# A delta-rule attention kernel: the look-ahead work of its first pass moved into the rounds of the second

## The chip, the cores and the metric

One core of a Trainium2 chip. The metric is the device time of the whole program in microseconds, lower is better. TensorE does matmuls into PSUM, VectorE (DVE) and ScalarE (ACT) move and combine tiles, GpSimd (POOL) works on SBUF tiles only, and SyncE (SP) issues most of the DMAs.

## The reference

Three stages follow each other: an attention with a running 40 x 40 state per head (4 batches, 8 heads, 768 tokens), a mixture of eight experts with one expert per token, and a dense layer. The change is in the first alone:

```python
for t in range(S):
    y[:, :, t] = einsum('bhd,bhde->bhe', rt, state)
    Sa = einsum('bhde,bhe->bhd', state, at)
    state = state * wt[:, :, None, :] - einsum('bhd,bhe->bhde', Sa, bt) + einsum('bhd,bhe->bhde', vt, kt)
```

## The kernel before

The attention works in chunks of C = 64 tokens. A step (or round) k takes one chunk of 8 pairs of heads; there are 24, twelve for one half of the batches and then twelve for the other, so the state is zero again after round 11. Within a chunk the effect of the a and b vectors on each other is a triangular matrix whose two 32 x 32 diagonal blocks are inverted; the lower left block (`off`) joins the halves later.

**First pass (24 steps).** For each step VectorE makes the decays of the chunk by two scans, `suf` backwards (L431) and `wq` forwards (L438) with a reciprocal between them (L436), and scales with them: `second` = b times suf (L445), `alpha` = a times wq (L446). TensorE makes from these the blocks (`g1`) and b turned to have time on the partitions (`bt`), each by `heads` (L764), 16 matmuls that the profile shows as 32 records. ScalarE copies the blocks to `off_all` and, negated, b to `btm_all` (L676 to L679). SP writes the blocks to memory in another order (L356) and loads them for the inversion (L294), with four steps in one group (GROUP), so 128 blocks of 32 x 32 lie on 128 partitions. Groups 0 and 1 are inverted by VectorE in halves of 16 (`invert_halves`, L130, behind step 11, AT_DVE), and the eight steps of these groups are then joined by small matmuls in steps 15 to 22 (AT_JOIN, L892 to L904). Groups 2 to 5 are inverted whole by GpSimd (`invert_blocks`, L109): two memsets, then for each of 31 columns j a product and a subtraction over (j+1)(31-j) elements per partition, each waiting for the one before.

**Second pass (24 rounds).** VectorE makes the same scans again (for k, the key) two rounds ahead, and `second` and `alpha` one round ahead. TensorE runs 17 groups by `heads` and one by `picks` per round inside a hardware loop (L916), each behind semaphores of what it reads: w (alpha with the state, and g2 with v), s (turned state), ktm, u, a part of the new state, z, m1, sa and sat, st (new state), m2, g2 of the next round, y. The banks are shared: w, z, sat and m2 lie in BA, s, m1 and y in BB, u, sa and g2 in BC, the key, the new state and the picks in BD. VectorE masks g2, m1 and m2 (L477), adds z to w (L517), scales the new state to `swt` (L534), takes y out of its bank (L452) and reduces the gate logits (L459). ScalarE takes out w, s, ktm, u, sa, sat, and prepares `off`, `btm`, `inv` (L708) for the next round. TensorE may write s only when y_out has read BB.

The order on each engine is written out by hand; each engine does its instructions in that order. SP's list per round is at L375 to L393. Around the loop stand warming matmuls (`warm`, L837). After the last round come the routing, the experts and the dense layer, which no edit touches.

Of the kernel before, what the change touches and what calls it, by code (L numbers as in the profile page):

```python
# [15 lines left out]
PARTS = 128  # L16
# [92 lines left out]
def invert_blocks(eng, sem, base, h, q, share):  # L109

    count = [0]
# [6 lines left out]
    link(eng.memset(flat, 0.0))  # L118
    link(eng.memset(flat[:, 0:B * B:B + 1], 1.0))
    for j in range(B - 1):  # L120
# [9 lines left out]
def invert_halves(eng, sem, h, q, share):  # L130

    count = [0]

    def link(ins):
        count[0] += 1
        ins.then_inc(sem, 1)
        eng.wait_ge(sem, count[0])

    def on_diagonal(t, i, j, rows_of, columns):
        first = t[:, B * i + j:B * i + j + 1]  # L140
        return bass.AP(first.tensor, first.offset, [first.ap[0], (HB * B + HB, 2 * BY_DVE), rows_of, columns])
    for j in range(HB - 1):
        n = HB - 1 - j
        part = share[:, 0:BY_DVE * 2 * (j + 1) * n].rearrange("q (d j t) -> q d j t", d=2 * BY_DVE, t=n)
        link(eng.tensor_tensor(part, on_diagonal(q, 0, j, (B, j + 1), (0, n)), on_diagonal(h, j, j + 1, (0, j + 1), (1, n)), ALU.mult))
        rest = on_diagonal(q, 0, j + 1, (B, j + 1), (1, n))
        link(eng.tensor_tensor(rest, rest, part, ALU.subtract))


HB = B // 2  # L150
HALVES_STEPS = 2 * (HB - 1)
INVERT_STEPS = 2 + 2 * (B - 1)
BLOCK_AT = B * B + B
BY_DVE, AT_DVE = 2, 11
JOINED = BY_DVE * GROUP
AT_JOIN = 15
BY_POOL = range(BY_DVE, GROUPS)


def attention(nc, inp, dram, keep):  # L160

    with ExitStack() as ctx:
# [3 lines left out]
        def ring(name, n, shape):  # L166
            return [m_.sb(f"{name}{s}", shape) for s in range(n)]
        W_COLS, A_COLS = HS * WIDE, HS * C
        t_in = ring("t_in", TR, [PARTS, W_COLS + 2 * A_COLS])
        restart = m_.sb("restart", [PARTS, HS, WIDE])  # L170
        suf = ring("suf", 2, [PARTS, HS, WIDE])
        wq = ring("wq", 3, [PARTS, HS, WIDE])
        wqx = ring("wqx", 2, [PARTS, HP, WIDE])
        alpha, second = (m_.sb(n, [PARTS, HS, C]) for n in ("alpha", "second"))
        ax = m_.sb("ax", [PARTS, HP, C])
        g1s = ring("g1s", 2, [PARTS, HS, B])
        off_all = m_.sb("off_all", [PARTS, STEPS, HS, B])
# [9 lines left out]
        blk, solved = (m_.sb(n, [PARTS, 2 * BLOCK_AT + B * B]) for n in ("blk", "solved"))  # L187
        share, share_dve = m_.sb("share", [PARTS, B * B // 4]), m_.sb("share_dve", [PARTS, BY_DVE * HB * HB // 2])
# [4 lines left out]
        late = m_.sb("late", [PARTS, 5 * ROUTE + NET * EXPERTS])  # L193

        def late_part(n, **sizes):
# [5 lines left out]
        joint = late[:, 0:JOINED * HS * HB].rearrange("q (k p t) -> q k p t", k=JOINED, p=HS)  # L201
        block_now = ring("block_now", 2, [PARTS, HS, B])
        turned_now = share_dve[:, :].rearrange("q (p t) -> q p t", p=HS)
        across_now = m_.sb("across_now", [PARTS, HS, HB])
# [9 lines left out]
        at_tile = t_in[1][:, 0:NTT * NETS].rearrange("q (t n) -> q t n", n=NETS)  # L214
        at_row_r, at_tile_r = m_.sb("at_row_r", [PARTS, NTT, ET], F32R), m_.sb("at_tile_r", [PARTS, NTT, NETS], F32R)
# [6 lines left out]
        LATE = 3  # L222
# [3 lines left out]
        first_f, running_f, place_f = (m_.sb(n, [PARTS, EXPERTS, LATE]) for n in ("first_f", "running_f", "place_f"))  # L226
        counted = m_.sb("counted", [PARTS, EXPERTS])
# [5 lines left out]
        s_wqx, s_inv_in, s_g1st = ([m_.sem(f"{n}{s}") for s in two] for n in ("s_wqx", "s_inv_in", "s_g1st"))  # L233
        s_blk, s_tt = ([[m_.sem(f"{n}{s}_{part}") for part in range(GROUP)] for s in range(3)] for n in ("s_blk", "s_tt"))
        s_ax_vtm, s_vt_rr = (m_.sem(n) for n in ("s_ax_vtm", "s_vt_rr"))
        s_step, s_step_dve = m_.sem("s_step"), m_.sem("s_step_dve")
        s_set, s_suf, s_rw, s_wq, s_wc, s_second, s_alpha1, s_alpha0, s_alpha = (m_.sem(n) for n in (
            "s_set", "s_suf", "s_rw", "s_wq", "s_wc", "s_second", "s_alpha1", "s_alpha0", "s_alpha"))
        names = ("turned", "across", "joint", "g1", "bt", "w", "s", "u", "ktm", "z", "m1", "sa", "sat", "st", "g2", "m2", "y", "pick")
# [7 lines left out]
        s_eye, s_patch, s_d1 = (m_.sem(n) for n in ("s_eye", "s_patch", "s_d1"))  # L247
        s_ready, s_choice = (m_.sem(n) for n in ("s_ready", "s_choice"))
        d1_now = [t[:, :, :].rearrange("q s e -> q (s e)")[:, 0:HS * HB].rearrange("q (s t) -> q s t", t=HB) for t in (w_tm, ktm)]
        block = ctx.enter_context(nc.Block())  # L250
        LASTS = {11: 4, 16: 12, 21: 20}

        def group_of(t, g):
            return t[:, BLOCK_AT * (g % 3):BLOCK_AT * (g % 3) + B * B].rearrange("q (j t) -> q j t", t=B)

        def block_of(k):
            return off_all[:, 2 * JOINED + k] if k < JOINED else g1s[k % 2][:, :, :]

# [11 lines left out]
        def _(sp):  # L270
            def load_t(j):
                if j >= TR:
                    if j - TR < STEPS:
                        sp.wait_ge(s_alpha1, j - TR + 1)
                    elif j - TR == STEPS:
                        sp.wait_ge(s_alpha0, 1)
                    else:
                        sp.wait_ge(s_alpha, j - TR - STEPS)
                src = inp["wab"][j] if j < STEPS else inp["wak"][j - STEPS]
                sp.dma_start(t_in[j % TR][:, :], src).then_inc(s_t[j % TR], 16)  # L280

            def solved_group(g):
                if g < BY_DVE:
                    sp.wait_ge(s_step_dve, HALVES_STEPS)
                else:
                    sp.wait_ge(s_step, INVERT_STEPS * (g - BY_DVE + 1))

            def load_blocks(j):
                g, n = j // GROUP, j % GROUP
                part = slice(4 * HS * n, 4 * HS * n + 4 * HS)  # L290
                sp.wait_ge(s_g1st[j % 2], 32 * turn(j))
                if g >= 3 and n == 0:
                    solved_group(g - 3)
# [1287 lines left out]
```

## Time and profile before

| | us |
|---|---|
| median of 3 runs | 1065.79 |
| the 3 runs | 1060.79 to 1067.89 |
| profiled execution | 1059.71 |
| its span | 1058.0 |
| TensorE busy | 953.2 |
| VectorE busy | 715.2 |
| ScalarE busy | 443.5 |
| GpSimd busy | 268.0 |

The span goes from the first to the last instruction of one profiled execution. Busy times are of the whole span; TensorE's matmuls are pipelined, so that its busy time holds waits inside the pipeline too. A matmul of `heads` takes some 0.2 us from start to end, but four run side by side on different parts of the array, so a group's time is read from the starts of neighbouring groups. A row of the timeline gives start, time, engine, line, operation, tiles, shape, count, and in brackets the idle time before it and what ended it.

### The profile page before, as it was taken

How to read it: one execution, taken by the hardware profiler on the slowest of the kernel's cores; microseconds unless marked ns; L12 is line 12 of the kernel's file. 1: busy time of each engine (PE TensorE's matmuls, PEld its weight loads, DVE VectorE, ACT ScalarE, POOL GpSimd, SP SyncE). 2: the span in 40 equal slices, each digit the busy share in tenths (PEclk: the TensorE clock that was granted, in tenths of full speed). 3: DMA queues.
4: the chain of work that ended last, by engine and by line, in shares of the span. 5: the costliest groups of instructions: out<-in, count | busy, mean ns of one | idle time of the engine just before them, and what ended most of it. 6: DMA issues, size and time to landing. Idle time of an engine off the chain costs nothing. (4 is left out here: it accounts for less than half of the span.)

```text
span 1058.0 us, 48713 instructions
## 1 busy us (share of the span) xinstructions
PE 953.2 (90%) x21425; PEld 873.0 (83%) x21425; DVE 715.2 (68%) x1122; ACT 443.5 (42%) x940; POOL 268.0 (25%) x348
## 2 busy tenths in 40 slices
PE   3426779999999998999999999879999999999997
PEld 2426769888888867998999999758899999999997
DVE  8997957898988763555555555567666565666654
ACT  5526635755565513555555555523221212222211
POOL 1009989798900004114111100140001000000000
PEclk9999977999999998999999999999999999999999
DMA  7968856988888637998586855130100101010100
GB/s 233 258 190 221 223 152 180 260 251 255 250 262 246 177 123 246 320 331 292 193 256 193 255 172 169 32 87 7 38 8 25 25 1 26 2 25 1 26 1 25
DMA packets 118354, 159.62 MB, mean 151 GB/s; under 512 B 68516, under 2 KB 87860, under 8 KB 117908
## 3 DMA queue, kind: packets, MB, share of 16 engines
q1 hardware_dynamic: 103956, 125.12, 39.5%
q0 software_dynamic: 5872, 25.28, 7.7%
q10 hardware_dynamic: 8464, 8.43, 2.5%
q8 instruction: 36, 0.59, 0.2%
q14 instruction: 26, 0.21, 0.1%
HBM read 133.15 MB, written 19.23 MB: 144 GB/s over the span
## 5 line engine op out<-in xcount | busy, mean ns | idle before, releaser
L1452 ACT CAST g_hi<-g 128x512 fp32r<-128x512 f32 x96 | 59.5, 620 | 278.1 <-DVE g L1396 274.5
L1305 PE MATMUL y_bank<-w_out_hi,g_hi 128*128 128x320 f32 x380 | 118.5, 312 | 5.0 <-DVE g_lo L1370 4.2
L1133 DVE TENSOR_TENSOR w_lo<-w_all,w_hi 128x640 fp32r<-128x640 f32 x124 | 102.0, 825 | 30.1 <-ACT w_hi L1173 24.3
L1093 PE MATMUL h_bank<-xt,w 128*128 128x128 f32 x992 | 121.0, 279 | 1.2 <-issue 0.9
L1093 PEld LDWEIGHTS h_bank<-xt,w 128*128 128x128 f32 x992 | 114.2, 192 | 6.0 <-issue 2.1
L1305 PE MATMUL y_bank<-w_out_hi,g_lo 128*128 128x320 f32 x380 | 117.7, 310 | 0.0
L1305 PE MATMUL y_bank<-w_out_lo,g_hi 128*128 128x320 f32 x380 | 117.5, 309 | 0.0
L1392 DVE TENSOR_SCALAR neg<-h_bank,slope 128x512 f32<-128x512 f32 x96 | 72.0, 750 | 65.9 <-PE h_bank L1292 62.3
L1292 PE MATMUL h_bank<-xt_hi,w_in_hi 128*128 128x512 f32 x288 | 113.5, 394 | 0.5 <-DVE xt_hi L1353 0.5
L1292 PE MATMUL h_bank<-xt_hi,w_in_lo 128*128 128x512 f32 x288 | 112.6, 391 | 0.0
L1370 DVE TENSOR_TENSOR g_lo<-g,g_hi 128x512 fp32r<-128x512 f32 x96 | 66.5, 692 | 65.8 <-ACT g_hi L1452 64.4
L1126 DVE SCALAR_TENSOR_TENSOR ht_lo<-h_bank,ht_hi 128x512 fp32r<-128x512 f32 x62 | 42.8, 691 | 88.3 <-ACT ht_hi L1166 86.3
L1173 ACT CAST w_hi<-w_all 128x640 fp32r x124 | 89.9, 727 | 27.9 <-PE y_bank L1105 20.3
L127 POOL TENSOR_TENSOR solved<-solved,share 128x31 f32<-128x31 f32 (+15 forms) x124 | 95.5, 770 | 9.7
L768 PE MATMUL bank<-alpha,second 40*64 40x64 f32 x1568 | 45.2, 270 | 58.3 <-DVE alpha L446 55.7
L124 POOL TENSOR_TENSOR share<-solved,blk 128x31 f32<-128x31 f32 (+15 forms) x124 | 92.7, 748 | 9.7
L768 PEld LDWEIGHTS bank<-alpha,second 40*64 40x64 f32 x1568 | 39.0, 179 | 61.7 <-issue 61.7
L95 POOL DMA_INDIRECT x<-x_rows_mid,order x31 | 31.6, 1018 | 200.0 <-DVE order L593 103.5
L1305 PEld LDWEIGHTS y_bank<-w_out_hi,g_hi 128*128 128x128 f32 x380 | 71.5, 188 | 10.4 <-DVE g_lo L1370 5.7
L1105 PE MATMUL y_bank<-w_hi,ht_hi 128*128 128x320 f32 x248 | 79.1, 319 | 0.0
L1166 ACT ACTIVATE ht_hi<-h_bank 128x512 fp32r<-128x512 f32 x62 | 37.1, 598 | 96.9 <-PE h_bank L1093 95.5
L1105 PE MATMUL y_bank<-w_lo,ht_hi 128*128 128x320 f32 x248 | 76.7, 309 | 0.0
(215 smaller groups left out, 2154.6 us busy)
## 6 DMA issues: line engine op xcount, KB each, us to landing
w<-w_in SPq DMA_DIRECT2D x31, 1024.0 KB
t_in<-wab_in SPq DMA_DIRECT2D x24, 776.0 KB, 4.7
t_in<-wak_in SPq DMA_DIRECT2D x24, 776.0 KB, 6.4
w_all<-w_in POOLq DMA_DIRECT2D x8, 1280.0 KB, 8.9
rr<-rr_in SPq DMA_DIRECT2D x24, 384.0 KB
w_rest<-w_in SPq DMA_DIRECT2D x62, 128.0 KB
vt<-vt_in SPq DMA_DIRECT2D x24, 256.0 KB
vtm<-vtm_in SPq DMA_DIRECT2D x24, 240.0 KB, 3.1
```

What stands on the lines that cost most here:

```text
L124: link(eng.tensor_tensor(part, q[:, 0:j + 1, j:j + 1].to_broadcast(shape), h[:, j:j + 1, j + 1:B].to_broadcast(shape), ALU.mult))
L127: link(eng.tensor_tensor(rest, rest, part, ALU.subtract))
L768: last = pe.matmul(out[HALF * to:HALF * to + rows_out, row, n * i:n * i + n], lhs, rhs, start=opens and i == 0, stop=closes and i == HP - 1)
L1093: last = pe.matmul(h_bank[s][h][:, f * ET:(f + 1) * ET], w1[s][:, k, (FH * h + f) * PARTS:(FH * h + f + 1) * PARTS], xt[s][:, k, :], start ...
L1105: last = pe.matmul(y_bank[s][:, 0:FEAT], h[s][:, f, :], w[:, f, :], start=f == 0 and n == 0, stop=f == NF - 1 and n == 2)
L1133: dve.tensor_tensor(piece(w2_lo, p), of_expert(e, p), piece(w2_hi, p).bitcast(F32), ALU.subtract).then_inc(s_w2lo, 1)
L1173: act.copy(piece(w2_hi, p), of_expert(e, p)).then_inc(s_w2hi, 1)
L1292: last = pe.matmul(h_bank[j % 2][:, :], w[:, k, f * PARTS:(f + 1) * PARTS], x_part[b % 2][:, k, :], start=n == 0, stop=n == len(passes) - 1)
L1305: last = pe.matmul(y_bank[n][:, 0:FEAT], g_part[j % RING][:, n * PARTS:(n + 1) * PARTS], v[:, f, :], start=f == 0 and p == 0, stop=f == NF ...
L1370: dve.tensor_tensor(g_lo[j % RING][:, :], g[j % 2][:, :], g_hi[j % RING][:, :].bitcast(F32), ALU.subtract).then_inc(s_glo, 1)
L1392: dve.tensor_scalar(neg[j % 2][:, :], h_bank[j % 2][:, :], 0.0, keep.slope[:, f:f + 1], ALU.min, ALU.mult).then_inc(s_neg, 1)
L1452: act.copy(g_hi[j % RING][:, :], g[j % 2][:, :]).then_inc(s_ghi, 1)
```

## The change

The first pass ends after twelve steps (AHEAD_OF = 12) of scans; the other twelve are made inside rounds 0 to 11 of the second pass, twelve steps ahead. `suf`, `wq`, `alpha`, `btm` and `off` of twelve steps are kept in rings, so the second pass no longer makes its own scans; the key is scaled by the kept `suf` (`scaled_key`), and the copy to the last column of `wq` is now made in each of the 24 steps. The g1 and bt groups of the step ahead go into bank BC beside u. There is no inversion in halves and no joining: group 0 is inverted whole by VectorE before step 8, groups 1, 2, 3 and 5 by GpSimd, group 4 by VectorE in six pieces in rounds 12 to 14. TensorE skips g1 and bt from the fourteenth pass of the loop on by two conditional branches. GpSimd stores its own inverses.

```diff
-BY_DVE, AT_DVE = 2, 11
-AT_JOIN = 15
+AHEAD_OF = STEPS // 2
+FIRST_BY_DVE, LATER_BY_DVE = 0, 4
+BY_POOL = (1, 2, 3, 5)
+AT_DVE = 8
+COLUMNS_AT = {12: ((0, 5), (5, 10)), 13: ((10, 15), (15, 21)), 14: ((21, 26), (26, 31))}
...
+            def store_blocks(k):
+                sp.wait_ge(out_of["g1"], k + 2)
+                blocks = dram["g1"][k].rearrange("(x p) f n j t -> x n j (p f) t", x=2)
+                for x in two:
+                    for n in two:
+                        first = HALF * x + B * n
+                        sp.dma_start(blocks[x, n], staged[k % 2][first:first + B, :, B * n:B * n + B]).then_inc(s_g1st[k % 2], 16)
...
+            for r in range(STEPS):
+                more, k, j = r + 1 < STEPS, r + 1, r + AHEAD_OF - 1
                 if more:
-                    cross_wq(k + 1)
-                if k >= 2:
-                    store_rows(k - 2)
+                    cross_wq(k)
+                if r == max(COLUMNS_AT) + 1:
+                    store_inverses(LATER_BY_DVE, 2)
+                if more and r >= 1:
+                    load_inverses(k)
+                if r + 2 < STEPS:
+                    load_k(r + 2)
+                if r >= 2:
+                    store_rows(r - 2)
                 if more:
-                    load_vtm(k + 1)
-                    load_vt(k + 1)
+                    load_vt(k)
+                if j < STEPS:
+                    store_blocks(j)
+                    if j % GROUP == GROUP - 1:
+                        load_blocks(j // GROUP)
                 if more:
-                    load_rr(k + 1)
+                    load_vtm(k)
+                    load_rr(k)
+                if j + 1 + TR < STEPS:
+                    load_t(j + 1 + TR)
...
+            for j in range(AHEAD_OF):
+                if j == AT_DVE:
+                    dve.wait_ge(s_blk[FIRST_BY_DVE], 16)
+                    invert_columns(dve, s_step_dve, 0, blocks_of(FIRST_BY_DVE), inverses_of(FIRST_BY_DVE), share_dve)
+                suffixes(j)
+                prefix_starts(j)
+                prefixes(j)
+                scaled(j)
+            scaled_key(0)
...
             for k in range(STEPS):
-                more = k + 1 < STEPS
+                more, j = k + 1 < STEPS, k + AHEAD_OF
                 if k >= 1:
                     y_out(k - 1)
...
-                if k + 2 < STEPS:
-                    suffixes(STEPS + k + 2)
-                if more:
-                    dve.wait_ge(did["ktm"], k + 1)
-                    scaled(STEPS + k + 1, s_alpha)
+                if j < STEPS:
+                    suffixes(j)
+                elif k in COLUMNS_AT:
+                    later_columns(k, 0)
+                dve.wait_ge(did["m1"], k + 1)
+                masked(m1, BB).then_inc(out_of["m1"], 1)
+                if j < STEPS:
+                    prefix_starts(j)
                 dve.wait_ge(did["z"], k + 1)
...
-                dve.wait_ge(did["m1"], k + 1)
-                masked(m1, BB).then_inc(out_of["m1"], 1)
+                if more:
+                    scaled_key(k + 1)
+                if j < STEPS:
+                    prefixes(j)
+                elif k in COLUMNS_AT:
+                    later_columns(k, 1)
...
                 if more:
                     dve.wait_ge(did["g2"], k + 2)
                     masked(g2, BC).then_inc(out_of["g2"], 1)
+                if j < STEPS:
+                    scaled(j)
...
+                invert_columns(pool, s_step, INVERT_STEPS * n, blocks_of(g), inverses_of(g), share)
+                pool.dma_start(in_memory(dram["tt"], g), inverses_of(g)).then_inc(s_tt[g], 16)
...
+                act.copy(btm[:, :, :].rearrange("q p e -> q (p e)"), btm_ring[:, k % AHEAD_OF].rearrange("q p e -> q (p e)"))
+                if k >= 1 and j < STEPS:
+                    keep_alpha(j)
...
+                if j < STEPS:
+                    stage_blocks(j, BC, BESIDE_U)
+                if more:
+                    alpha_for(k + 1)
                     cross_alpha(k + 1)
...
+                if j < STEPS:
+                    keep_btm(j, BC, BESIDE_U)
+                    keep_off(j)
...
-                heads(turned(second), BD, DIM, done="ktm")
+                heads(turned(key), BD, DIM, done="ktm")
+                with pe.If(i < AHEAD_OF + 2):
+                    g1_product(i + (AHEAD_OF - 1), BC, BESIDE_U)
                 arrive(out_of["w"], i)
                 heads(u_product, BC, DIM, done="u")
+                arrive(s_vt_rr, 32 * i)
                 arrive(out_of["s"], i)
+                heads(m1_product, BB, C, done="m1")
                 arrive(out_of["ktm"], i)
-                heads(from_s(lambda i, q, m: eye(m)), BD, DIM, closes=False)
-                heads(from_k(lambda i, q, m: at_m(vtm, i, q, m, rows(m))), BD, DIM, opens=False, closes=False)
+                heads(from_k(lambda i, q, m: at_m(vtm, i, q, m, rows(m))), BD, DIM, closes=False)
                 arrive(out_of["u"], i)
                 heads(low_part, BA, DIM, done="z")
-                arrive(s_vt_rr, 32 * i)
-                heads(m1_product, BB, C, done="m1")
+                heads(from_s(lambda i, q, m: eye(m)), BD, DIM, opens=False, closes=False)
+                arrive(out_of["m1"], i)
+                heads(from_k(lambda i, q, m: m1[rows(m), slot(q, i), :]), BB, C, closes=False)
+                with pe.If(i < AHEAD_OF + 2):
+                    arrive(out_of["g1"], i + AHEAD_OF)
+                    bt_product(i + (AHEAD_OF - 1), BC, BESIDE_U)
...
-                arrive(s_alpha, i)
-                heads(with_alpha(second), BC, C, done="g2")
-                heads(from_k(lambda i, q, m: m1[rows(m), slot(q, i), :]), BB, C, opens=False, closes=False)
+                arrive(out_of["bt"], i + AHEAD_OF)
+                arrive(s_key, i + 1)
+                arrive(s_now, i + 1)
+                heads(with_alpha(key, alpha_now), BC, C, done="g2")
```

## Rows read from the trace of the kernel before

**Rows 1.** Stages: length, busy PE, PEld, DVE, ACT, POOL, clock, DMA share, GB/s.
```profile
65.30:137.50 72.20, 49.38 (x2414) 43.89 (x2414) 64.94 (x72) 38.77 (x121) 56.07 (x57) 1.00 0.82 215
137.50:187.00 49.50, 42.89 (x2168) 41.01 (x2172) 31.90 (x52) 22.85 (x60) 44.20 (x69) 0.76 0.60 173
187.00:377.40 190.40, 178.79 (x11520) 168.42 (x11516) 160.87 (x297) 111.46 (x274) 92.38 (x132) 1.00 0.79 235
```
**Rows 2.** Timeline of VectorE, a step of the first pass without GpSimd.
```profile
24.93 0.68 DVE L446 TENSOR_TENSOR alpha<-t_in,wq 128x512 f32<-128x512 f32 x1
25.53 1.25 DVE L431 TENSOR_TENSOR_SCAN suf<-t_in,restart 128x528 f32<-128x528 f32 x1
...
29.56 1.25 DVE L431 TENSOR_TENSOR_SCAN suf<-t_in,restart 128x528 f32<-128x528 f32 x1
```
**Rows 3.** Timeline of VectorE, the inversion in halves: its start, widest instructions and end.
```profile
53.81 0.21 DVE L145 TENSOR_TENSOR share_dve<-solved,blk 128x60 f32<-128x60 f32 x1
...
59.06 0.42 DVE L145 TENSOR_TENSOR share_dve<-solved,blk 128x256 f32<-128x256 f32 x1
59.52 0.42 DVE L147 TENSOR_TENSOR solved<-solved,share_dve 128x256 f32<-128x256 f32 x1
...
65.31 1.26 DVE L431 TENSOR_TENSOR_SCAN suf<-t_in,restart 128x528 f32<-128x528 f32 x1
```
**Rows 4.** Timeline of VectorE and GpSimd, first pass, GpSimd inverting.
```profile
104.02 0.94 DVE L445 TENSOR_TENSOR second<-t_in,suf 128x512 f32<-128x512 f32 x1
104.49 1.00 POOL L127 TENSOR_TENSOR solved<-solved,share 128x252 f32<-128x252 f32 x1
104.89 1.16 DVE L446 TENSOR_TENSOR alpha<-t_in,wq 128x512 f32<-128x512 f32 x1
...
105.58 0.98 POOL L124 TENSOR_TENSOR share<-solved,blk 128x255 f32<-128x255 f32 x1
```
**Rows 5.** Timeline, a round of the second pass without GpSimd.
```profile
320.83 0.32 DVE L534 TENSOR_TENSOR swt<-bank,wq 128x160 f32<-128x160 f32 x1
...
321.91 0.68 DVE L477 TENSOR_TENSOR g<-bank,later 128x512 f32<-128x512 f32 x1
...
322.43 0.66 PE L768 MATMUL bank<-m,btm 64*40 64x64 f32 x32
...
323.14 0.42 DVE L452 TENSOR_TENSOR yt<-bank,wq 128x256 f32<-128x256 f32 x1 [0.55 <-PE bank L768]
323.38 0.22 PE L768 MATMUL bank<-swt,alpha 40*64 40x40 f32 x1 [0.29 <-issue]
...
330.29 0.32 DVE L534 TENSOR_TENSOR swt<-bank,wq 128x160 f32<-128x160 f32 x1
```
**Rows 6.** Timeline of the first rounds, and one stretch of them (columns as rows 1).
```profile
144.71 0.36 PE L768 MATMUL bank<-vtm,ktm 64*40 64x40 f32 x4 [3.85 <-issue]
...
150.61 0.32 DVE L534 TENSOR_TENSOR swt<-bank,wq 128x160 f32<-128x160 f32 x1 [0.84 <-PE bank L768]
...
153.20 0.35 PE L768 MATMUL bank<-alpha,second 40*64 40x64 f32 x8 [1.80 <-issue]
...
155.62 0.30 PE L768 MATMUL bank<-swt,alpha 40*64 40x40 f32 x1
...
170.20 0.30 PE L768 MATMUL bank<-swt,alpha 40*64 40x40 f32 x1
...
187.04 0.32 DVE L534 TENSOR_TENSOR swt<-bank,wq 128x160 f32<-128x160 f32 x1
...
153.00:171.00 18.00, 17.80 (x713) 17.47 (x716) 11.05 (x17) 6.60 (x17) 16.35 (x22) 0.53 0.53 160
```
**Rows 7.** Timeline: a store of blocks on SP's queue, the first pass's last alpha.
```profile
24.97 1.26 SPq L356 DMA_DIRECT2D g_mid<-off_all  x2
...
131.00 1.07 DVE L446 TENSOR_TENSOR alpha<-t_in,wq 128x512 f32<-128x512 f32 x1
```

More of the change, by code:

```diff
@@ L106, with invert_columns @@
 COMBOS = ((0, 0), (0, 1), (1, 0), (1, 1))
-def invert_blocks(eng, sem, base, h, q, share):
-    count = [0]
+def invert_columns(eng, sem, base, h, q, share, first=0, last=B - 1):
+    count = [0 if first == 0 else 2 + 2 * first]
     def link(ins):
@@ L117, in invert_blocks @@
     flat = q.rearrange("q j t -> q (j t)")
-    link(eng.memset(flat, 0.0))
-    link(eng.memset(flat[:, 0:B * B:B + 1], 1.0))
-    for j in range(B - 1):
+    if first == 0:
+        link(eng.memset(flat, 0.0))
+        link(eng.memset(flat[:, 0:B * B:B + 1], 1.0))
+    for j in range(first, last):
         n = B - 1 - j
@@ L127, in invert_blocks @@
         link(eng.tensor_tensor(rest, rest, part, ALU.subtract))
[L130 to L151, printed above, removed]
 INVERT_STEPS = 2 + 2 * (B - 1)
 BLOCK_AT = B * B + B
-BY_DVE, AT_DVE = 2, 11
-JOINED = BY_DVE * GROUP
-AT_JOIN = 15
-BY_POOL = range(BY_DVE, GROUPS)
+AHEAD_OF = STEPS // 2
+FIRST_BY_DVE, LATER_BY_DVE = 0, 4
+BY_POOL = (1, 2, 3, 5)
+SOLVED_IN = (0, 1, 0, 1, 1, 0)
+SOLVED_BEFORE = {2: 0, 3: 1, 4: 3, 5: 2}
+AT_DVE = 8
+BESIDE_U = HP * C
+COLUMNS_AT = {12: ((0, 5), (5, 10)), 13: ((10, 15), (15, 21)), 14: ((21, 26), (26, 31))}
 def attention(nc, inp, dram, keep):
@@ L369, in _ @@
                     load_vtm(0)
                     load_vt(0)
[L371 to L393 removed]
+                    load_rr(0)
@@ L838, in warm @@
                 for _ in range(count):
-                    pe.matmul(BB[:, 0, 0:HS * DIM], keep.ones[:, :], btm_all[:, 0].rearrange("q p e -> q (p e)"), start=True, stop=True)
+                    pe.matmul(BB[:, 0, 0:HS * DIM], keep.ones[:, :], btm_ring[:, 0].rearrange("q p e -> q (p e)"), start=True, stop=True)
             pe.wait_ge(s_bank, 1)
             pe.wait_ge(s_const, 4)
-            def quarter(b):
-                return slice(B * b, B * b + B)
-            def blocks(product, out, rows_out, n, done):
-                for p in range(HP):
-                    for c in two:
-                        for b in range(4):
-                            lhs, rhs = product(b, slot(c, p))
-                            last = pe.matmul(out(c, p)[B * b:B * b + rows_out, :], lhs, rhs, start=p == 0, stop=p == HP - 1)
-                last.then_inc(did[done], 1)
@@ L869, in across, with g1_product @@
-            def across(s):
-                def product(b, p):
-                    part, other = crossed_to(b, p)
-                    return block_now[s][part, other, :], turned_now[part, other, 0:HB]
-                return product
-            def joint_half(s):
-                return lambda b, p: (across_now[quarter(b), p, :], d1_now[s][quarter(b), p, :])
-            def g1_product(count):
+            def g1_product(count, out, at):
                 arrive(s_alpha1, count)
                 arrive(out_of["g1"], count)
-                heads(with_alpha(second), BA, C, done="g1")
```

403 lines of the change are left out of this document (161 added, 242 removed).

## The prediction

> **What bounds the kernel now.** I cut the span into stages first [rows 1]. Up to 137.5 us a first pass of 24 steps runs; from there to 377.4 us the 24 rounds of the second pass; what follows (routing, experts, dense layer) has the same code in both kernels and is left alone. In the first pass VectorE sets the pace: it is busy 64.9 of the 72.2 us from 65.3 to 137.5, TensorE 49.4. One step is one turn of VectorE's five instructions: the suffix scans of two neighbouring steps start 4.03 us apart [rows 2]. In the second pass TensorE is busy 178.8 of 190.4 us and VectorE 160.9 [rows 1], so TensorE bounds, with VectorE close behind. A round takes 9.46 us (the new states are written at 320.83 and 330.29 [rows 5]). In records, 11520 over 32 is 360 groups of 32 (one call of heads or picks each), 18 per round, at 178.79/360 = 0.497 us each [rows 1].
>
> Two more things matter here. GpSimd and VectorE take turns when both read two SBUF tiles: the alpha product takes 0.68 us alone [rows 2] and 1.16 beside GpSimd, and one VectorE and one GpSimd instruction alternate, 1.09 us for the pair [rows 4]. And the first rounds lose time: TensorE stops 3.85 us before 144.71 and 1.80 us before 153.20 with "issue" as the cause, the granted clock is 0.53 from 153 to 171 us, that is mostly the lower level of 1.2 GHz, and round 1 takes 170.20 - 155.62 = 14.6 us [rows 6]. Rounds 0 to 3 take from 137.5 to the state write at 187.04; at 9.46 a round, and 6.9 us from a round's start to its state write (330.29 - 323.38 [rows 5]), that would be 35.3 us. The loss is 14.3 us.
>
> **The change, part by part.**
> (a) First pass, steps 0 to 7. A step gains the copy that was only in the second pass (a small one, some 0.2 us), so 4.25 us. Five steps back from 25.53 [rows 2] the first scan starts at 5.4 us; eight steps end at 39.4.
> (b) Whole inversion of group 0 on VectorE. Before, 30 instructions on halves take 65.31 - 53.81 = 11.5 us, and the widest (256 columns) follow each other at 59.52 - 59.06 = 0.46 [rows 3]. The sizes are 4(j+1)(15-j), 5440 columns in all, so an instruction costs 0.186 us plus 0.00107 per column. Whole blocks need 62 instructions over 2 x 5456 = 10912 columns: 11.5 + 11.7 = 23.2, plus 1.2 for two memsets, 24.4 us. GpSimd joins on the way: the blocks of step 7 leave TensorE near 41; four stores now go out in SP's order at 0.63 each (two took 1.26 [rows 7]), and the landing, the load of the group and its landing some 6 us more. So GpSimd starts near 50, with 38 of VectorE's 62 instructions left. A VectorE instruction of 256 columns holds the port some 0.30, GpSimd's of 252 some 0.49 (1.09 less 0.6 for the 512-column product): 0.79 instead of 0.46 in the worst pairing, 0.33 more. Bounds: 0 (no collision) and 38 x 0.33 = 12.5. GpSimd's first columns are small, so I take 6.5. The inversion ends at 39.4 + 24.4 + 6.5 = 70.3.
> (c) Steps 8 to 11 beside GpSimd: its reads add 0.48 us to an alpha product, 0.26 to the pitch of second and 0.4 or so to a scan [rows 2, 4]: 5.3 a step, 5.65 with the copy. 22.6 us, to 92.9. Then the key product, the first g2, the warming matmuls; before, 5.4 us lie between the last alpha's end at 132.07 [rows 7] and the loop. With the key in front 6.1: the loop starts at 99, against 137.5. Gain 38.5. It carries the removed twelve steps and all joining, less the whole inversion.
> (d) First round. It should lose as before does, for the same loop is entered cold: warm 7.6 us to the state write, plus 7. Bound below: no loss. Above: one further stop and one more slow round, 9 us.
> (e) Rounds 1 to 11. TensorE gets two more groups per round (g1 and bt), 2 x 0.497 = 1.0 us, and two conditional branches, which no row shows; the loop's own backward branch leaves a gap of 0.48 between the last group (322.43 + 0.47) and 323.38 [rows 5], so each branch lies between 0 and 0.5; taken 0.1, nearest to nothing because the branch falls through to the next instruction. The old groups do not shrink, but four waits are better covered by the new order, so 20 groups are 10.0. The new wait is VectorE's: the scalings of the step ahead (second, alpha) now stand behind g2 and in front of y_out, and TensorE cannot write s before y_out has read its bank. Counted from the state write: g2's mask starts 1.08 later [rows 5], then 0.61 each for g2, second, alpha and 0.76 for y_out (two of 0.42 [rows 5]), 3.7 us. TensorE is at that wait after 2.55 (323.38 - 320.83) less one group moved away, plus two groups, 3.0. It waits 0.7 alone and, with 0.8 for the scalings beside GpSimd, 1.5. GpSimd works in some seven of the twelve rounds. Round: 10.0 + 1.0 = 11.0. Behind TensorE's wait queue s, ktm, g1 and u, and so the whole round. ScalarE's additions (staging, two alpha copies, off, about 2.2 us a round) lie beside TensorE's groups; ScalarE comes to some 9.9 of 11 us, so this cover is thin: below 10 us a round it would bind. SP has 6.5 us of issues a round, with vtm and rr now behind four block stores, some 2.5 us late; vtm lands about when alpha_s wants it, inside the y wait. The DMA carries 256 KB of k and the blocks more; its share of 0.79 [rows 1] goes to about 0.9. Bounds of a round: 10.1 (no wait) and 12.0 (wait 1.5 and half a microsecond of late DMA). Eleven rounds are 121, and the slow clock after the first round adds 8, as before (36.4 us from 150.61 to 187.04 against 28.4 [rows 6]): 129.
> (f) Rounds 12 to 14, where VectorE inverts group 4. No scans and no scalings any more; the rest is 4.4 us a round (starts follow each other some 0.07 sooner than the durations say: state 0.47, two masks at 0.61, m1 0.65, y 0.76, gates 0.2, add 0.49, key 0.65), 13.2, plus 1.2 for the scaling behind round 11. The columns take 24.4. The blocks of step 23 arrive near the end of round 12, so GpSimd inverts group 5 beside the other 42 instructions: 0 to 42 x 0.33 = 14, taken 9, as its small columns come first. VectorE alone fills 47.8 us; TensorE's 9 to 10 us per round lie beside it. I take 48.3.
> (g) Round 15: the long idle stretches before may leave TensorE at 1.2 GHz. A slow round took 14.6 [rows 6]. 0 to 5.5 lost, taken 3.5: 12.5. Rounds 16 to 23: 18 groups, 8.95, with the branches 9.05; eight make 72.4.
> Sum: 99 + 14.6 + 129 + 48.3 + 12.5 + 72.4 = 375.8 for the last state write, against 377.4. The change gives 38.5 and takes back 36.9: -1.6 us. The profiled execution took 1059.71 us (span 1058.0 plus 1.7); the median of the runs is 1065.79, 6.1 above it. On the median: 1064.2. A measurement of this kernel tells about 1% (10.7 us) from no change.
>
> **A rule against this change.** In the rows the loop of 18 groups, more than 1150 matmul and load instructions, jumps back for 0.48 us, and only the first time through are there stops of 3.85 and 1.80 us [rows 5, 6]. The Trainium skill (Runtime: NRT & Kernel Launch, section Instruction fetch mechanics) says that instructions are prefetched in sequence alone, and that a taken branch to a page outside the two held must wait for a fetch; by the trace the backward branch does not pay that, so the rule's price is seen here at first entry only.
>
> **The rivals.**
> R1, faster: the round is TensorE's alone. If y_out's wait is hidden (VectorE's pitches slightly shorter, TensorE's groups slightly longer) rounds 1 to 11 take 10.2, 9 us less, and if the shorter straight code lets the first round run without stops and at full clock, another 15. For: 0.7 us is a small wait; the first-pass loop enters this one with little code between. Against: VectorE had under 0.6 us of slack a round already. 1064 - 24 = 1040.
> R2, slower: TensorE stays at 1.2 GHz longer. Place: rounds 1 to 5, where it now waits each round, and rounds 15 to 17 behind idle stretches. Price: a slow early round has 20 groups, 14.6 x 20/18 = 16.2, 5.2 over 11.0; a late one 5.5. For: the slow clock held from 153 to 171 us though TensorE was busy 17.80 of the 18 [rows 6], so it does not come back at once. Against: it never fell from 187 to 377 us [rows 1]. It decides from 2.4 slow rounds beyond those counted; with five it is 1064 + 26 = 1090.
> R3, slower: the skipped branches of the last eleven rounds each stop TensorE for a fetch: 22 skips at 1.80 to 3.85 us [rows 6] are 40 to 85 us, 1104 to 1149. Against: the jump is over some 64 instructions only, and the far jump back is cheap. This is what the skill's rule named above would do if the target were outside.
> R4: the change does not shorten the first pass as stated, since the inversion and GpSimd collide at the upper bounds (6 us more in b, 5 in f) and rounds take 11.5: 1064 + 16 = 1080. I count it with R2's side.
>
> **How the numbers follow.** Forecast (within 1%) 0.36; R1 0.34; R2 and R4 together 0.25; R3 0.05. The range reaches from below R1 (rounds at the lower bound without the collisions, 1036) to above R2 (1092); R3 stays outside with part of the tails. Faster by over 1% 0.34, within 1% 0.36, slower by over 1% 0.30. Inside the forecast's own case the range is 1055 to 1075.
>
> **What would show it.** The loop's first matmul near 99 us; state writes 11.0 apart in rounds 1 to 11 with TensorE idle before s, put down to y_out; VectorE's column instructions in rounds 13 and 14 at up to 0.8 us instead of 0.46; rounds 16 to 23 at 9.05. Wrong if the loop starts after 105, if rounds are under 10.4 or over 12, if the slow clock covers more than three rounds, or if "issue" stands before u or sa in the late rounds.

## The result and the profile after

| | before | after |
|---|---|---|
| median of 4 runs, us | 1063.76 | 1105.46 |
| the 4 runs, us | 1060.79 to 1067.89 | 1099.2 to 1108.18 |
| span of the profiled execution, us | 1058.0 | 1097.5 |
| mean granted clock of TensorE | 0.982 | 0.939 |

The kernel is slower: the ratio is 1.039 (95% interval 1.0342 to 1.0438). The prediction was 1064.0, in the range 1036 to 1092. The profiled execution of the kernel after was the shortest of its four.

The windows view of the kernel after, cut at the state writes (`swt`, now L527, one at the end of each round); the columns are those of [rows 1]. In order: group 0's inversion, steps 8 to 11, round 0, rounds 1 to 5, round 9, round 10, round 14, rounds 16 to 23, and all that follows.

```profile
38.60:71.40 32.80, 1.95 (x64) 1.83 (x64) 30.51 (x65) 1.83 (x4) 20.70 (x37) 1.00 0.20 59
71.40:97.70 26.30, 13.11 (x247) 9.69 (x250) 22.88 (x27) 9.21 (x20) 24.34 (x26) 1.00 0.71 193
97.70:113.80 16.10, 11.26 (x523) 10.64 (x518) 3.23 (x6) 5.94 (x15) 3.68 (x11) 0.71 0.53 170
113.80:131.10 17.30, 16.70 (x651) 16.34 (x649) 9.52 (x15) 5.59 (x14) 15.42 (x25) 0.50 0.53 145
131.10:143.00 11.90, 10.42 (x640) 9.74 (x635) 9.94 (x16) 6.91 (x17) 10.96 (x13) 0.97 0.71 204
143.00:158.90 15.90, 14.36 (x651) 13.79 (x654) 9.59 (x16) 8.19 (x21) 13.51 (x23) 0.68 0.68 182
158.90:170.10 11.20, 10.23 (x640) 9.48 (x636) 8.34 (x16) 6.91 (x17) 0.00 (x0) 0.99 0.89 259
170.10:189.10 19.00, 15.34 (x649) 14.95 (x653) 8.89 (x16) 8.28 (x21) 12.14 (x24) 0.66 0.64 182
...
228.10:248.60 20.50, 14.91 (x653) 14.53 (x657) 8.38 (x17) 7.88 (x20) 0.00 (x0) 0.67 0.63 185
248.60:259.80 11.20, 10.18 (x644) 9.43 (x636) 8.31 (x17) 7.37 (x18) 0.00 (x0) 1.00 0.58 145
...
303.20:322.10 18.90, 14.69 (x576) 14.08 (x576) 17.28 (x30) 5.92 (x14) 16.86 (x27) 0.57 0.33 87
...
336.00:411.50 75.50, 72.47 (x4617) 68.18 (x4617) 38.11 (x86) 45.54 (x109) 0.00 (x0) 1.00 0.58 164
411.50:1097.50 686.00, 662.68 (x4551) 600.14 (x4549) 397.55 (x605) 239.36 (x408) 69.57 (x72) 0.99 0.35 110
```

Two kinds of round stand side by side with the same number of TensorE instructions (640 to 657). At a clock of 0.97 to 1.00 a round takes 11.2 to 12.0 us, near the forecast of 11.0; at 0.50 to 0.68 it takes 15.65 to 20.4. Rounds 1 to 11 were 17.3, 11.9, 15.9, 11.2, 19.0, 12.0, 15.65, 11.4, 20.4, 11.2 and 11.5, together 157.5 us: six good ones (69.2) and five slow ones (88.3).

State write by state write, against [rows 1, 6]: the first is 36.8 us earlier (113.81 for 150.61), which is what the change buys. Rounds 1 to 11 cost 43.5 more than before's eleven (157.5 for 114.0), rounds 12 to 14 22.9 more, round 15 4.5 more, rounds 16 to 23 the same (75.45 for 75.49). The last state write is at 411.48 for 377.38. The rest takes 686.0 for 680.6.

What stands in front of a slow round, in the timeline of the kernel after (L756 and L818 are TensorE's matmuls of groups and picks; the lines of [rows 5, 6] answer to these). "Alpha's group" is the first group of a pass, `swt,alpha_now`:

```profile
104.09 0.47 PE L756 MATMUL bank<-vtm,ktm 64*40 64x40 f32 x25 [2.77 <-issue]
...
113.00 0.70 PE L756 MATMUL bank<-sa_tm,x 64*40 64x40 f32 x28 [1.35 <-issue]
...
145.12 1.01 DVE L426 TENSOR_TENSOR second<-t_in,suf_all 128x512 f32<-128x512 f32 x1
...
146.05 1.07 DVE L429 TENSOR_TENSOR alpha_new<-t_in,wq 128x512 f32<-128x512 f32 x1
...
147.05 0.41 DVE L441 TENSOR_TENSOR yt<-bank,wq 128x256 f32<-128x256 f32 x1
...
147.94 0.50 PE L756 MATMUL bank<-eye,swt 40*40 40x40 f32 x30 [1.15 <-DVE yt L441]
...
148.27 0.65 PE L756 MATMUL bank<-eye,key 40*64 40x40 f32 x31
...
148.96 1.13 PE L756 MATMUL bank<-alpha_new,second 40*64 40x64 f32 x32
...
166.58 2.29 SPq L278 DMA_DIRECT2D g_mid<-w_rest  x4
...
171.41 0.34 SPq L287 DMA_DIRECT2D blk<-g_mid  x1
171.79 0.44 SPq L307 DMA_DIRECT2D vtm<-vtm_in  x1
...
176.05 0.26 PE L756 MATMUL bank<-swt,alpha_now 40*64 40x40 f32 x1 [3.57 <-DMA vtm<-vtm_in]
...
235.98 0.29 PE L756 MATMUL bank<-swt,alpha_now 40*64 40x40 f32 x1 [5.49 <-DMA vtm<-vtm_in]
...
303.90 1.10 PE L818 MATMUL bank<-pick,yt 40*64 40x48 f32 x32 [6.50 <-DVE swt L527]
```

Three causes can be read. In round 3, `second` and `alpha_new` take 1.01 and 1.07 us beside GpSimd, y leaves its bank at 147.8, and TensorE waits 1.15 us in front of s. The next group still runs at full pace (0.65 for 31), and from 148.96 on most take 1.1 instead of 0.68, to 159 us: the granted clock of 149 to 159 us is 0.50, with TensorE busy all of those 10.00 us. In rounds 5 and 9 SP first stores the last blocks of a group (166.58), waits for them to land so that it may load them (171.41), and only then issues `vtm` of the round (171.79); TensorE stands for 3.57 and 5.49 us. In round 13 VectorE does two pieces of columns in front of the state write of 303.20, and TensorE stands for 6.50 us. The waits view sums these pauses; their own total is 24.7 us, where rounds 1 to 15 lost 70.9 against before:

```profile
PE bank L756 <- DMA vtm<-vtm_in: 9.7, 3, 5.5
PE bank L818 <- DVE swt L527: 8.8, 2, 6.5
PE bank L756 <- DVE yt L441: 6.2, 9, 1.1
```

### The profile page after: what moved, and what is told of

It reads as the page before. It is cut to its first block and busy times, and to the rows that moved or that the text cites. A ratio compares the mean times of both kernels' runs of the same rounds, so it can differ in the third digit from the quotient of the medians.

```text
span 1097.5 us, 45432 instructions
## 1 busy us (share of the span) xinstructions
PE 962.8 (88%) x19825; PEld 882.1 (80%) x19825; DVE 677.3 (62%) x1124; ACT 427.7 (39%) x844; POOL 239.1 (22%) x350
## 5 line engine op out<-in xcount | busy, mean ns | idle before, releaser
L1236 PE MATMUL h_bank<-xt_hi,w_in_hi 128*128 128x512 f32 x288 | 113.6, 394 | 0.5 <-DVE xt_hi L1297 0.5
L128 POOL TENSOR_TENSOR solved<-solved,w 128x31 f32<-128x31 f32 (+15 forms) x124 | 81.7, 659 | 9.7
L756 PE MATMUL bank<-alpha_new,second 40*64 40x64 f32 x768 | 23.7, 285 | 68.4 <-DVE alpha_new L429 67.9
L1249 PEld LDWEIGHTS y_bank<-w_out_hi,g_hi 128*128 128x128 f32 x380 | 71.5, 188 | 10.5 <-DVE g_lo L1314 5.7
L125 POOL TENSOR_TENSOR w<-solved,blk 128x31 f32<-128x31 f32 (+15 forms) x124 | 77.7, 626 | 9.7
L756 PEld LDWEIGHTS bank<-alpha_new,second 40*64 40x64 f32 x768 | 20.4, 190 | 70.4 <-issue 69.2
L1049 PE MATMUL y_bank<-w_hi,ht_lo 128*128 128x320 f32 x248 | 76.6, 309 | 0.0
L1236 PE MATMUL h_bank<-xt_lo,w_in_hi 128*128 128x512 f32 x192 | 76.2, 397 | 0.0
```

The lines of the kernel that those rows point to most:

```text
L756: last = pe.matmul(out[HALF * to:HALF * to + rows_out, row, at + n * i:at + n * i + n], lhs, rhs, start=opens and i == 0, stop=closes and ...
L1049: last = pe.matmul(y_bank[s][:, 0:FEAT], h[s][:, f, :], w[:, f, :], start=f == 0 and n == 0, stop=f == NF - 1 and n == 2)
L1236: last = pe.matmul(h_bank[j % 2][:, :], w[:, k, f * PARTS:(f + 1) * PARTS], x_part[b % 2][:, k, :], start=n == 0, stop=n == len(passes) - 1)
L1249: last = pe.matmul(y_bank[n][:, 0:FEAT], g_part[j % RING][:, n * PARTS:(n + 1) * PARTS], v[:, f, :], start=f == 0 and p == 0, stop=f == NF ...
```

## The experiments

The theory, A: what was lost is TensorE's clock. A pause in the loop is followed by a stretch at 1.2 GHz, and it costs more by that than by its own length. The pauses have three causes: the load of a group ahead of `vtm` on SP, VectorE's scalings in front of y, VectorE's columns in rounds 12 to 14. The rivals: the rounds are long because VectorE, SP or the DMA has too much to do, whatever the clock; or they are long by TensorE's own count of work. In the expectations these are theory B. Each experiment edits the kernel after.

The executions of one kernel, with the same work, already differ by the clock: those of the kernel after took 1099.2, 1105.3, 1105.6 and 1108.2 us at mean clocks of 0.939, 0.936, 0.932 and 0.927, and those of the kernel with filler below come in the same order. So the stages that are read below from one profiled execution each can fall a little differently in the next one, and the medians are given beside them.

**The group's load behind vtm.**

```diff
-                    if j % GROUP == GROUP - 1:
-                        load_blocks(j // GROUP)
                 if more:
                     load_vtm(k)
                     load_rr(k)
+                if j < STEPS and j % GROUP == GROUP - 1:
+                    load_blocks(j // GROUP)
```

> SP issues vtm and rr of the next round before the load of a group's blocks, nothing else. Theory A (the clock: a pause of TensorE makes the granted clock fall to 1.2 GHz for most of the next round, and that is the larger part of the loss): the pauses of 3.57 us before round 5 and 5.49 us before round 9 vanish, and with them part of what the rounds behind lose (19.0 and 20.4 us against 11.2 to 12); 9 us of waiting plus 0 to 16 us of slow clock, the lower end if the wait for y alone makes the clock fall there too, as it does before rounds 3 and 7. Theory B (the added work and the port, the clock is a by-product): 9 us less and no more. Against the changed kernel (1105): A 1082 to 1096, B 1096.

Measured: 1086.69 us, ratio to before 1.021 (1.0145 to 1.0276), 18.8 us under the kernel after. SP's timeline and round 5 of this kernel:

```profile
168.38 1.98 SPq L278 DMA_DIRECT2D g_mid<-w_rest  x4
170.40 0.46 SPq L307 DMA_DIRECT2D vtm<-vtm_in  x1
...
173.23 0.33 SPq L287 DMA_DIRECT2D blk<-g_mid  x1
```

```profile
170.40:182.10 11.70, 10.11 (x640) 9.43 (x641) 8.41 (x16) 7.48 (x19) 4.60 (x9) 1.00 1.00 299
```

Round 5 falls from 19.0 to 11.8 us, though its wait for `vtm` shrank only from 3.57 to 1.34: the other 5.0 went with the slow clock. Round 9 falls from 20.4 to 11.2. Round 5 is this short with the DMA at a share of 1.00, so the DMA's load alone does not make a round slow. Rounds 2, 3, 7 and 8 are slow behind pauses for y of 0.97 to 1.15 us (14.5 to 15.8), and round 10 behind one of 1.69 us for `vtm` (16.0). Rounds 2, 8 and 10 were good before this edit, so rounds 1 to 11 together give back only 6.7 us (150.8 for 157.5). The median lies in A's range and under B's 1096; the profiled execution alone, at 1089.86 us 9.3 under that of the kernel after, does not tell the two apart.

**Scalings and the first g1 later.** Scalings of the step ahead go behind y_out and the gates, g1 behind z; ScalarE copies alpha right behind `btm`, and prepares the next alpha before it stages blocks.

```diff
                 if j < STEPS:
-                    scaled(j)
...
+                if k >= 1 and j - 1 < STEPS:
+                    scaled(j - 1)
                 if j < STEPS:
                     suffixes(j)
```

> VectorE scales the step ahead behind y_out instead of in front of it, g1 goes behind z on TensorE and its alpha copy behind u on ScalarE; the late vtm stays. Theory A: TensorE's wait of 0.4 to 1.2 us for y_out goes in rounds 1 to 11 (some 8 us), the clock no longer falls before rounds 3 and 7, so these two take 11 instead of 15.9 and 15.7 us: 16 to 18 us less in all, 1087 to 1089. Theory B: 8 us less, 1097. If the wait only moves to g1 or bt, about 1100 to 1105 by both.

Measured: 1096.39 us, ratio 1.0336 (1.0282 to 1.039). Its rounds 3 and 4 in windows, and what its waits view lists for TensorE in front of s and alpha's group:

```profile
139.70:155.80 16.10, 14.16 (x656) 13.78 (x660) 10.39 (x17) 8.08 (x21) 14.49 (x21) 0.68 0.81 227
155.80:166.50 10.70, 9.99 (x652) 9.44 (x646) 8.42 (x17) 7.29 (x19) 3.13 (x9) 1.00 0.72 211
```

```profile
PE bank L757 <- DMA vtm<-vtm_in: 17.5, 6, 7.4
```

The waits for y are gone from the view and a good round takes 10.5 to 10.8 us instead of 11.2 to 12. But TensorE now comes to alpha's group sooner and waits there for the DMA instead: 17.5 us in six waits for 9.7 in three. Rounds 3 and 7, which A expected at 11 us, take 16.2 and 16.4 behind waits of 1.85 and 2.15 us for `vtm`. What one cause gave up, the next largely took. By its time this run lies where B put it (1097, against 1087 to 1089 for A), so it does not speak for A by itself.

**Group 4 on GpSimd.** No columns on VectorE in rounds 12 to 14.

```diff
-BY_POOL = (1, 2, 3, 5)
+BY_POOL = (1, 2, 3, 4, 5)
...
-COLUMNS_AT = {12: ((0, 5), (5, 10)), 13: ((10, 15), (15, 21)), 14: ((21, 26), (26, 31))}
+COLUMNS_AT = {}
```

> GpSimd inverts group 4 too, VectorE has no columns in rounds 12 to 14. Rounds 12 to 14 took 14.0, 18.2 and 18.9 us (state write to state write from 271 to 322) and round 15 13.9 at the lower clock. By both theories they become 9.5 to 10.5 each if GpSimd is done with group 4 by round 15 and with group 5 by round 19: 51 + 13.9 becomes 40, 25 us less, 1080. If GpSimd is late, it shows as waits for inv_in at rounds 16 or 20, and 1090 to 1100. Rival: without VectorE's columns the time only moves to lower clock elsewhere, 1095.

Measured: 1085.66 us, ratio 1.0194 (1.0122 to 1.0266), 19.8 us under the kernel after. From state write 11 (279.56) to state write 15 (325.80) it takes 46.2 us for 64.7 (271.30 to 336.03). But GpSimd now works beside rounds 10 and 11 too, and they take 15.85 and 14.7 us for 11.2 and 11.5, behind waits of 1.08 and 1.25 us for y, and round 13 16.0, behind 3.06 for `vtm`. The time stays 5.7 us above the 1080 expected:

```profile
269.69 0.50 PE L754 MATMUL bank<-eye,swt 40*40 40x40 f32 x30 [1.25 <-DVE yt L439]
...
296.22 0.30 PE L754 MATMUL bank<-swt,alpha_now 40*64 40x40 f32 x1 [3.06 <-DMA vtm<-vtm_in]
```

**Work for TensorE in the pause.** The same waits, but four matmuls on constants in front of the wait for y, into a part of bank BC that nobody reads.

```diff
+                for _ in range(4):
+                    pe.matmul(BC[:, 0, BESIDE_U:BESIDE_U + PARTS], keep.ones[:, :], keep.upper[:, :], start=True, stop=True)
                 arrive(out_of["y"], i)
                 heads(turned_state, BB, DIM, done="s")
```

> Nothing of the order changes; TensorE gets four more matmuls of 128 columns on constants in each round, in front of its wait for y, some 0.96 us of added work a round. Their result is not used. Theory A: TensorE no longer pauses there, so the clock stays up before rounds 3 and 7 (and perhaps comes back sooner elsewhere): 10 us less for these two rounds, and 0.5 us more in the rounds with a short wait or none (some 8 us over 16 rounds): 1095 to 1105, with fewer stretches at 0.50 in the windows. Theory B: the added work costs 0.5 to 1 us in each round, 1112 to 1125, with the clock as before.

Measured: 1110.02 us, ratio 1.0456 (1.0378 to 1.0533). Rounds 3 and 7 of this kernel:

```profile
148.50:160.50 12.00, 11.37 (x652) 10.54 (x653) 9.13 (x17) 7.56 (x19) 10.44 (x18) 1.00 0.80 216
205.00:217.00 12.00, 11.40 (x652) 10.57 (x653) 9.61 (x17) 7.58 (x19) 10.98 (x14) 1.00 0.82 223
```

```profile
152.20 1.16 PE L860 MATMUL bank<-upper,ones 128*128 128x128 f32 x8
153.28 0.52 PE L756 MATMUL bank<-eye,swt 40*40 40x40 f32 x32
```

This is the sharpest of the tests for A. No useful instruction is moved, and GpSimd's, VectorE's and the DMA's work is unchanged; TensorE only does useless work where it stood. Rounds 3 and 7 take 12.0 us at full clock, where the kernel after took 15.9 and 15.65 at 0.68. What it does not separate is the filled pause from the kind of filler: these are 128x128 matmuls, and no run fills the pause with small ones. The filler costs about 1.2 us a round (late rounds 10.7 for 9.43), more than these two rounds give back, and it does not cover the wait for `vtm` (5.21 us in round 9), so the kernel as a whole is no faster. Its time lies between the two ranges, 1095 to 1105 for A and 1112 to 1125 for B; the rounds speak for A, the sum for neither.

**vtm ahead of the stores too.** SP's order is vtm, block stores, rr, group load.

> SP issues vtm of the next round ahead of the four block stores, and a group's load behind rr; nothing else. Theory A (the clock falls behind a pause, whatever ended it): no wait for vtm is left; the pauses for y of about 1 us stay and still drop the clock in two to four rounds, so 1080 to 1088, a little under the kernel where only the group's load was moved (1087). Theory C (the late vtm alone drops the clock, the wait for y does not): rounds 1 to 11 at 11.2 to 12 throughout, 1072 to 1076.

Measured: 1076.62 us, ratio 1.0218 (1.0124 to 1.0311). No wait for `vtm` is left. Four of the rounds 1 to 11 are slow: 17.0 for the first, and 14.6 to 15.7 for rounds 4, 7 and 8, each behind a pause for y (0.99, 1.34 and 0.93 us). So a late `vtm` is not needed for a slow round, against C, though the time itself fell just below A's range and just above C's. Pauses of 0.85, 0.91 and 0.86 us in rounds 2, 3 and 6 were followed by nothing.

**vtm first and group 4 on GpSimd.**

> As the one above, and GpSimd inverts group 4 as well. Theory A: the columns' 22 us come off as far as the wait for y leaves the clock up in rounds 10 to 14, where GpSimd now works: 1062 to 1075. Theory C: 1050 to 1056.

Measured: 1066.01 us over 10 runs, ratio 1.0055 (1.0009 to 1.0102). Its waits view:

```profile
PE bank L755 <- DVE yt L440: 10.7, 11, 1.4
PE bank L755 <- DMA vtm<-vtm_in: 0.5, 1, 0.5
```

GpSimd now works in all of rounds 1 to 12, the wait for y stands in eleven places, and in six of them it is over 1 us (two in the kernel after). The profiled execution, at 1072.06 us, was the longest of the ten. In it rounds 1 to 11 take 156.3 us (114.09 to 270.35), against 142.9 with `vtm` first alone (111.46 to 254.37): 13.4 us are given back here of the 18.6 that rounds 12 to 15 gained.

**All three: vtm first, scalings later, group 4 on GpSimd.**

> Three moves together: vtm ahead of the block stores, the scalings behind y_out (with g1 behind z), group 4 on GpSimd. Theory A: neither pause is left, so after the first two rounds the clock stays up, rounds 2 to 11 at 10.6 to 10.8, rounds 12 to 23 at 9.4: last state write at 97.7 + 15 + 17 + 107 + 113 = 350, against 377 in the kernel before, in all 1036 to 1042, that is 2% under it. Theory B (added work and the shared port are the cost): rounds 2 to 11 at 11.5 or more, 1060. A further wait that shows up only now (ax, rr, inverses) would give 1045 to 1060 and its name.

Measured: **1050.36 us** over 10 runs (1045.53 to 1056.7), where the kernel before ran at 1058.58 beside it; ratio 0.994 (0.9904 to 0.9976). Its stages, rounds 1 to 11, 12 to 15, 16 to 23 and the rest:

```profile
112.50:250.40 137.90, 123.07 (x7044) 116.95 (x7037) 106.15 (x175) 82.27 (x196) 111.91 (x165) 0.89 0.77 218
250.40:289.20 38.80, 36.98 (x2368) 34.76 (x2368) 20.45 (x41) 25.66 (x63) 33.87 (x62) 1.00 0.74 198
289.20:364.20 75.00, 71.85 (x4613) 67.87 (x4617) 38.33 (x85) 46.20 (x111) 18.85 (x34) 1.00 0.64 178
364.20:1048.50 684.30, 661.36 (x4551) 600.73 (x4550) 397.62 (x605) 239.44 (x408) 70.76 (x72) 0.98 0.35 111
```

With the pauses of y and of the columns removed, the same computation in the same look-ahead scheme is faster than the kernel after, by 55 us in the medians and by some 48 (an estimate) by the ratios, 1.039 to 0.994, since the kernel before ran 5 us lower beside this one. It is 0.6% under the kernel before, which is less than the 1% that the prediction calls no change. Rounds 12 to 15 come down from 64.7 to 38.8. The further wait that the expectation allowed for is that for `vtm` at alpha's group: 8.4 us in six rounds. Rounds 1, 3 and 10 are still slow (17.3, 14.3 and 15.3), the last two behind waits of 1.55 and 1.47 us there. But round 6, behind the longest of the six, is not:

```profile
181.07 0.22 PE L756 MATMUL bank<-swt,alpha_now 40*64 40x40 f32 x1 [1.61 <-DMA vtm<-vtm_in]
```

```profile
177.50:189.10 11.60, 9.66 (x630) 9.10 (x621) 9.59 (x16) 7.16 (x18) 10.43 (x16) 1.00 0.91 264
```

**Loads and scalings without group 4.** The combination before, with the columns on VectorE again.

> The kernel after with vtm first and the group's load last on SyncE, and with the scalings behind y_out, the gates and the reordered ScalarE work, but VectorE still inverting group 4 in rounds 12 to 14. Theory A (what was lost is TensorE's granted clock, and each pause has its own cause): the three parts add up. Loads first alone took 28.8 us off the time of after, loads first with group 4 on GpSimd 39.4, all three 55.1 (1105.5 - 1050.4), so the missing scalings are worth 15.7 and this kernel should come to 1076.6 - 15.7 = 1061 us, with rounds 1 to 11 near 10.7 apiece where the clock stays at 2.4 GHz and rounds 12 to 14 as in the kernel after, near 50 us together. Rival (each part removes the same pause, the parts overlap): no better than the better of the two, 1075. Either way the state writes of rounds 0 to 11 should be those of the kernel with all three parts within 3 us.

Measured: 1075.4 us, ratio 1.0104 (1.0041 to 1.0167). State write 11 came at 250.05 (250.41 with all three), and then 63.1 us pass to state write 15, where all three take 38.8. The state writes between lie up to 5.9 us apart, not within 3, and the slow rounds are 1, 6 and 8 instead of 1, 3 and 10. The sum did not come out as A said: 1061 was expected, and the rival's 1075 came. In the traces the parts are not independent: group 4 on GpSimd brings state write 15 forward by 23.9 us when the scalings stand behind y (313.19 to 289.25) and by 2.6 when they stand in front of it (316.91 to 314.32), where it lengthens the pauses for y. The times bear this out less clearly. The medians give 25.0 and 10.6 us, but the ratios to the kernel before, which ran beside each, fall by 0.016 both times (1.0104 to 0.994, and 1.0218 to 1.0055), and the interval of `vtm` first alone spans some 20 us. How far the parts depend on each other stays open.

**Alpha's copy ahead of the staging.** All three parts, and:

```diff
                 if more:
                     alpha_for(k + 1)
+                    cross_alpha(k + 1)
...
                     stage_blocks(j, BC, BESIDE_U)
-                if more:
-                    cross_alpha(k + 1)
```

> All three parts (1050.4 us), and on ScalarE the cross copy of alpha for the next round is issued ahead of the staging of the blocks instead of behind it, some 0.4 us earlier. Theory: TensorE's wait at alpha_s (1.55, 1.28, 1.18 and 1.47 us in four rounds) is for whichever of vtm and alpha's copy lands last; if it is the copy, the waits shrink to under 1.0 and up to four rounds come back from 14 to 10.6 us, 1036 to 1048 us in all. Rival: it is vtm, or the DMA's own 3.7 to 5 us of landing, and the time is 1050 within 5 us.

Measured: 1054.29 us over 9 runs, ratio 0.9939 (0.9901 to 0.9978): no gain over 1050.36, and within the rival's 1050 give or take 5. The waits for `vtm` at alpha's group sum to 6.3 us in seven places for 8.4 in six; in rounds 3, 8, 9 and 10 they are 0.93, 1.02, 1.36 and 0.95 us for 1.55, 1.28, 1.18 and 1.47, so the copy was part of it but not all. Two rounds are slow, 1 and 6 (17.0 and 15.1 us), instead of three, but rounds 5 and 9 take 13.0, and rounds 1 to 11 together 136.6 us for 137.9. Which of `vtm` and the copy lands last in each round stays open, since one semaphore counts both.

## Why the prediction was wrong

(a) to (d), the first pass and the first round: the sum was right, in part by luck. The inversion ended at 71.3 (70.3 predicted), the loop's first group came at 97.7 (99), state write 0 at 113.81 (113.6). Inside it the inversion took 32.7 us for 30.9 and the first round 16.2 for 14.6, against 2.0 less for steps 8 to 11 and an inversion that began 0.8 sooner. The collision of [rows 4] is there: a column of this width takes 0.27 us alone and 0.70 beside GpSimd. Over the inversion, by the same count of 24.4 us without it, it cost 8.3 us and not the 6.5 taken:

```profile
41.28 0.27 DVE L125 TENSOR_TENSOR w<-solved,blk 128x112 f32<-128x112 f32 x1
...
65.97 0.70 DVE L125 TENSOR_TENSOR w<-solved,blk 128x112 f32<-128x112 f32 x1
...
71.10 0.21 DVE L128 TENSOR_TENSOR solved<-solved,w 128x31 f32<-128x31 f32 x1
```

(e), rounds 1 to 11, is the step that failed: 129 us predicted, 157.5 measured, 28.5 of the 41 by which the profiled execution missed (1099.2 for 1058.1). The wait for y, 0.7 alone and 1.5 beside GpSimd, was real and smaller (0.42, and up to 1.15); the round itself, 11.0, was a little short of the 11.5 that the six good ones take on average, 5.9 us over eleven. Wrong was the term for the slow clock: "the slow clock after the first round adds 8, as before". I had given the clock to the entry of the loop alone and let the new wait for y cost only its own length. The five slow rounds lie 30.6 us above five good ones; 9.1 of that are the waits for `vtm`, and the other 21.5 stand where the sum has 8. The second error stands in the same step: "vtm lands about when alpha_s wants it, inside the y wait". Four block stores were counted in front of it; that SP waits behind them for their landing, so as to load the group, was not, although the line stands in the change. With the loads moved, round 5 fell by 7.2 us; filler in the pause for y took rounds 3 and 7 down by 3.9 and 3.7.

(f), rounds 12 to 14, 48.3 predicted, 50.8 measured: VectorE's sum was nearly right, since there VectorE is the bound: busy 46.8 us where 47.8 were counted. (g), round 15, 12.5 and 13.9: mis-sized by 1.4. Rounds 16 to 23 were put at 9.05 each and took 9.43, as before's same eight (9.44). No gain from the new order shows there; the stop in front of alpha's group is still 0.29, as in [rows 5]:

```profile
376.30 0.22 PE L756 MATMUL bank<-swt,alpha_now 40*64 40x40 f32 x1 [0.29 <-issue]
```

That is 3.0 us. The stages behind the rounds, taken as unchanged, are 5.4 longer; half of that, 2.7, lies ahead of the first gathered rows, which VectorE copies 34.0 us behind the last state write for 31.3 (its wait for them is 9.24 us for 7.79, and the one before it 4.42 for 3.63). No run tested it; with all three parts it is 684.3, with a different last stretch of SP's work.

The rivals. R2, TensorE longer at 1.2 GHz, is what happened; its price (5.2 us for an early slow round) fits a slow round with a short pause (15.65 to 17.3, against 11.5). Its count is near: it allowed for five beyond those in the sum, and beyond round 1, which the sum had, there were rounds 3, 5, 7 and 9, and round 14 at 0.57. Its place (rounds 1 to 5) does not fit: 3, 5, 7 and 9 each lie behind a pause. To this come 9.1 us of waits for `vtm`, which belonged to no rival. R1's pitch of 10.2 was reached nowhere; the nearest is 10.5 to 10.8, with the scalings later. R3 did not occur: the stops put down to "issue" in rounds 2 to 11 are 0.16 to 0.37 us, and rounds 16 to 23, with two skips each, take what before's take. R4's collision in the inversion was 1.8 us larger than taken, where the rival had 6. Of the prediction's own signs two fell: "if the slow clock covers more than three rounds", and rounds "over 12".

The clock itself: the Trainium skill (TensorE: Matmul & The Clock Gate, Part 1) gives two levels and sets them by how busy TensorE has been of late. The levels agree with the rows, 0.50 and 1.00 in those of the kernel after. That a TensorE busy for 10.00 of 10 us stays at 0.50 does not follow from the rule as it stands there; the groups are of small matmuls (40x40 to 64x64) and the filler's are 128x128, and no run separates size from idle time. What decides whether the clock falls stays open.

## What to carry to other kernels

When a change adds a wait to a loop that TensorE bounds, look at the clock before the sum: price a pause of a microsecond by the stretch at half clock that may follow (here some 4 us), not by its own length, and list every queue that can make one. Work that is moved into a loop goes behind the instruction that releases TensorE, on VectorE, ScalarE and the DMA queue alike, and a load that waits for its own kernel's stores goes last on its queue. Removing one pause alone can move the wait to the next one: the scalings later alone gave 9 us, and the three parts together 55 in the medians.

## What was not expected of the hardware

A pause of 1.15 us in a loop where TensorE is otherwise nearly always at work was followed, one microsecond later, by ten microseconds at half clock, and the same place with filler kept the full clock. It is not a sure thing, and the length of the pause does not decide it: in the same kernel 0.90 us (round 7) was followed by it, and 0.83 us (round 2), 1.10 (round 6) and 0.55 (round 8) were not; nor were 1.61 us with all three parts (round 6) and 1.36 in the last kernel (round 9). What decides between them stays open.

And the granted clock of the profile can miss a slow stretch. Round 1 of the last kernel (alpha's copy first) took 17.0 us at a shown clock of 1.00. The window of its round 1, and the same group in its rounds 1 and 3:

```profile
113.70:130.70 17.00, 16.40 (x651) 16.04 (x648) 8.70 (x15) 6.16 (x15) 9.49 (x20) 1.00 0.66 178
```

```profile
121.00 1.10 PE L755 MATMUL bank<-w_tm,inv 64*64 64x40 f32 x32
...
146.58 0.68 PE L755 MATMUL bank<-w_tm,inv 64*64 64x40 f32 x32
```

The groups ran at the pace of 1.2 GHz (1.10 for 0.68 us), so this kernel's mean clock of 0.984 is too high. The length of a known group is the surer clock.
